# An unused buffer of 1,408 bytes ahead of the streamed buffers of a convolution and two MLPs

## What is computed

```
out  = einsum('hk,bskhg->bshg', softmax(weight), windows(x))   # 7 taps
h    = x @ w_in                                                # MLP 1
g    = where(h >= 1, h, where(h <= -1, 0, (h + 1)**2 / 4))
x    = g @ w_out
h    = x @ moe2_w_in                                           # MLP 2
out  = (h / (1 + exp(-1.702 * h))) @ moe2_w_out
```

## Time and profile before

| What | Value |
|---|---|
| Median of three runs | 1178.54 us |
| The profiled execution, its own time | 1179.53 us |
| Its span (first to last instruction) | 1177.8 us |
| Mean granted clock of TensorE | 0.993 |
| Busy: TensorE, its weight loads | 97%, 87% |
| Busy: VectorE, ScalarE, GpSimd | 70%, 68%, 36% |

### The profile page before, as it was taken

The page is one execution under the profiler, slowest core; times in us unless marked ns, Lnnn a source line. Parts: engine busy times, 40 slices in busy tenths (PEclk is TensorE's granted clock), DMA queues, the critical chain, the costliest instruction groups (busy, mean ns, idle before and its releaser), DMA issues.

```text
span 1177.8 us, 25920 instructions
## 1 busy us (share of the span) xinstructions
PE 1146.4 (97%) x9382; PEld 1021.9 (87%) x9382; DVE 820.4 (70%) x1206; ACT 795.8 (68%) x1510; POOL 429.1 (36%) x425
## 2 busy tenths in 40 slices
PE   7999889999999999999999999999999999999998
PEld 4768679989989999889988999888988988899987
DVE  6877557677676867767677686767767676676633
ACT  4866476776867677686776767677676766765554
POOL 5892909053170714508062260804408062000000
PEclk9999989999999999999999999999999999999999
DMA  6312010001010010100001010010101000000001
GB/s 192 97 40 71 2 35 15 35 3 47 1 48 1 10 40 1 48 1 15 35 5 44 1 48 2 12 37 1 48 1 48 1 7 9 2 15 3 14 1 28
DMA packets 63857, 31.27 MB, mean 27 GB/s; under 512 B 56084, under 2 KB 60562, under 8 KB 63760
## 3 DMA queue, kind: packets, MB, share of 16 engines
q1 hardware_dynamic: 63760, 29.80, 9.5%
HBM read 23.09 MB, written 6.29 MB: 25 GB/s over the span
## 4 chain that ended last, share of the span: by engine, by line
PE 71%; ACT 11%; issue 6%; DVE 6%; POOL 5%; DVEq 0%; ACTq 0%; POOLq 0%
ACT raw L986 3%; ACT clip L936 3%; DVE gate L1103 3%; PE acc_all L748 3%; PE acc_all L762 2%; PE acc_all L754 2%; PE acc_all L757 2%; PE acc_all L759 2%; PE acc_all L765 2%; PE h_all L697 2%; PE h_all L699 2%; PE h_all L701 2%; PE h_all L692 2%; PE h_all L695 2%; PE acc_all L738 2%
## 5 line engine op out<-in xcount | busy, mean ns | idle before, releaser
L1109 DVE TENSOR_TENSOR g_lo<-gate,g_hi 128x512 fp32r<-128x512 f32 x232 | 190.0, 819 | 153.0 <-ACT g_hi L942 153.0
L942 ACT ACTIVATE g_hi<-gate 128x512 fp32r<-128x512 f32 x232 | 146.5, 632 | 201.0 <-DVE gate L1103 199.4
L1115 DVE TENSOR_TENSOR g_lo<-h_all,g_hi 128x512 fp32r<-128x512 f32 x256 | 175.0, 684 | 117.7 <-ACT h_all L953 115.8
L950 ACT ACTIVATE g_hi<-h_all 128x512 fp32r<-128x512 f32 x256 | 152.9, 597 | 87.1 <-PE h_all L703 58.1
L508 POOL TENSOR_TENSOR x_conv<-x_in,tap_w 128x384 f32<-128x384 f32 (+1 forms) x29 | 24.8, 875 | 508.8 <-ACT raw L986 506.5
L936 ACT ACTIVATE clip<-clip,half 128x512 f32<-128x512 f32 x256 | 184.3, 720 | 34.8 <-DVE clip L1094 32.6
L1094 DVE TENSOR_SCALAR clip<-h_all 128x512 f32<-128x512 f32 x256 | 174.8, 683 | 23.5 <-PE h_all L701 19.9
L508 POOL TENSOR_TENSOR prod<-x_in,tap_w 128x384 f32<-128x384 f32 (+1 forms) x174 | 181.2, 1065 | 4.2
L515 POOL TENSOR_TENSOR x_conv<-x_conv,prod 128x384 f32<-128x384 f32 (+1 forms) x174 | 179.8, 1055 | 1.6
L1103 DVE TENSOR_TENSOR gate<-h_all,clip 128x512 f32<-128x512 f32 x232 | 159.3, 687 | 19.5 <-ACT clip L936 8.7
L953 ACT ACTIVATE h_all<-h_all 128x512 f32<-128x512 f32 x256 | 151.6, 592 | 0.1
(11 more groups left out here) (281 smaller groups left out, 4766.0 us busy)
## 6 DMA issues: line engine op xcount, KB each, us to landing
x_in<-in_x SPq DMA_DIRECT2D x14, 960.0 KB, 4.8
out_y<-raw SPq DMA_DIRECT2D x360, 16.0 KB, 1.4
raw<-in_moe_w_out SPq DMA_DIRECT2D x6, 384.0 KB, 4.0
raw<-in_moe_w_in SPq DMA_DIRECT2D x4, 512.0 KB, 3.8
raw<-in_moe_w_in SPq DMA_DIRECT2D x8, 256.0 KB, 4.5
stage<-in_moe_w_out SPq DMA_DIRECT2D x2, 384.0 KB, 7.5
x_in<-in_x SPq DMA_DIRECT2D x1, 768.0 KB, 11.0
x_in<-in_x SPq DMA_DIRECT2D x2, 283.5 KB
```

The lines of the kernel that those rows point to most:

```text
L942: nc.scalar.activation(g1_hi[step.s % G_RING][:, :], gate1_of(step)[:, :], ACT.Copy).then_inc(g1_hi_ready, 1)
L950: nc.scalar.activation(g2_hi[step.s % G_RING][:, :], src, ACT.Gelu_apprx_sigmoid).then_inc(g2_hi_ready, 1)
L1109: nc.vector.tensor_tensor(g1_lo[k][:, :], gate1_of(step)[:, :], g1_hi[k][:, :].bitcast(FP32), ALU.subtract).then_inc(g1_lo_ready, 1)
L1115: nc.vector.tensor_tensor(g2_lo[k][:, :], bank2(step)[:, :], g2_hi[k][:, :].bitcast(FP32), ALU.subtract).then_inc(g2_lo_ready, 1)
```

## The change

A buffer that nothing reads or writes is allocated between x_conv and x_set. Every buffer allocated after it moves up by 352 x 4 = 1,408 bytes; those before it stay. No instruction is added or taken away.

```diff
@@ -80,6 +80,8 @@
         x_blocks = [raw[0][:, 0:TT], raw[0][:, TT:2 * TT]]
         x_turned = [raw[1][:, 0:TT], raw[1][:, TT:2 * TT]]
 
+
+        sb("pad", [P, 352])
         x_set = [[sb(f"x_{k}_{side}", [P, TT], FP32R) for k in ("hi", "lo", "rest")] for side in "ab"]
         y_set = [[sb(f"y_{k}_{side}", [P, TT], FP32R) for k in ("hi", "lo", "rest")] for side in "ab"]
         y_part = sb("y_part", [P, TT])
```

## The result

The changed kernel took 1190.9 us (1190.42 to 1191.46, four runs) against 1178.72 us for the kernel before (1177.29 to 1179.02, four runs). The ratio is 1.0105, 95% interval 1.009 to 1.012: 12.2 us slower, outside the forecast's range and five times what a measurement can tell from nothing. The profiled execution of the changed kernel took 1190.42 us, with a span of 1188.7.

The account below looks back on a forecast made before the run. The prediction took TensorE's matmul rate as the bound. Between a 68 us gain and a 28 us loss it took 0 for the address, and zero for other engines and first loads: 1178.5 us, range 1174.5 to 1181.5 us.

Parts of the forecast that it names:

- What bounds the kernel: Whole kernel: TensorE is busy 97% of the span, so only the rate at which matmuls follow each other matters.
- Where the buffers lie: Streamed x, y and g buffers start 640 above a multiple of 2,048 before and at 0 after; weights stay.
- Rival E: Allocator's origin or order differs from the arithmetic, so the change doesn't do what it says; 1178.5 us, chance inside 0.73.
- the tail's four alignments: Second MLP's last tile: w_down streams at 128, 1,664, 1,152 and 640 above a multiple of 2,048, all 175 ns; taken as 0.
- crossings of 2,048 bytes: Streams read by TensorE: crossing a multiple of 2,048 bytes was taken to cost zero.
- The rule of the skill: Operand starts of 640 and 0 are both multiples of the 16-byte cacheline, so the sum stays at 0.
- rival D: TensorE's matmuls: next weight load runs into this stream, up to 232.5 ns a pair, 28 us slower, 1206 us; chance 0.10.
- Rivals A and B: A: stream's start costs the 13.6 ns, 1111 us, chance 0.06; B: same, but weight loads bind next, 1140 us, chance 0.05.
- the 13.6 ns: Paired matmuls at full clock: time per pair beyond the columns, 226.9 ns against 213.3 ns for 512 columns.
- Rival C: Slots of pairs: only irregular spacings get better, 20 ns x 232 = 5 us faster, 1173.9 us; chance 0.06.
- Other engines: ScalarE and VectorE on the moved buffers: 50 ns a slot at most, inside their free time, so nothing.
- the first loads: Moved stage buffers carrying the first w_out chunks: zero, with 1 us as the bound upwards.

Follow-up runs that it names:

- the maps: Four kernels with the computation left out, only matmuls at one placing of weights and stream after another; 226.7 ns a matmul settled at distance 0.

## Why the prediction was wrong, point by point

- **What bounds the kernel** was right: nothing but the rate of the matmuls moved, and it moved the whole time.
- **Where the buffers lie** was right as far as the runs can tell: the sums of sizes give the distances, and every kernel with another padding came out by them. With the origin of 16,512 that the maps' kernels write down, x_hi of side a lies at 16,512 + 147,968 = 164,480, which is 80 x 2,048 + 640, and the shift makes it 81 x 2,048. No trace shows an address. Rival E is out, since the time moved.
- **The step that failed** is the sentence "Between these ends I take 0, since the tail's four alignments are the nearest rows to the question and differ by nothing". It put the unknown term at nothing, and the runs showed 5.4 ns a pair, 12.2 us, in its place. All four have the weights at the stream's own remainder by 256, distance 0. Rows that vary the alignment by 512, 1,024 and 1,536 are four times the same case, so they spoke on crossings of 2,048 bytes, where they were right (with everything moved the streams cross none, and the time stayed), and on nothing finer. They also stream 384 columns, where the map has a price of 2.7 ns for distance 128 and not 6. The prediction saw that no stream started on a multiple of 512, and still gave the finer rules 0.27 of the chance.
- **The rule of the skill.** The prediction set "SBUF — State Buffer" of the Trainium skill beside its 0: a start's alignment there is a matter of legality, and the cacheline has 16 bytes. The section says that its runs timed nothing, so it never spoke for 0, and the prediction read too much into it. Nor is a line of 16 bytes the unit of the price: in the maps 4 bytes cost 12 ns. The part Who interferes with whom of that page of the Trainium skill was named against rival D. It speaks of ports between engines, and the map agrees that no other engine is needed. It also has stream and weight load on two independent ports; here, all the same, the spacing changed by 6.6 ns with the distance between the two.
- **Rival D** was what happened: it named the place, the distance of 128, the sign, and 0.228 to 0.233 us for a pair, where 0.2314 and 0.2333 were found. Its chance of 0.10 was far too small. The argument against it, that one weight slice in four starts at the streams' 640, failed like the tail's: by 256 all four slices are at distance 0. Its price was over twice the measured one, 28 us against 12.2, because it let all 4,984 matmuls pay and none of the waits shrink. Part pay already: the 232.5 ns after L754 in the earlier trace rows follow no idle time that the trace shows, and in the median the ten acc_all pairs of a slot took 2.299 us before instead of 10 x 226.7 = 2.267. And 10.8 us of weight-load waits were there to be used up; the prediction looked at the matmuls' waits only, the 0.2 us of L740 in the earlier trace rows, where the loads waited 3.6.
- **Rivals A and B** fall: with x, y and g on multiples of 2,048 and the weights moved along, the time is that of before. So the 13.6 ns aren't a head thrown away, and the match of 32 columns with 128 bytes meant nothing.
- **Rival C** came out with the other sign: at the new distance nearly every spacing is longer, the regular ones of h_all too (2.096 us for nine pairs instead of 2.040).
- **Other engines** and **the first loads** at nothing: nothing shows against it. The list of waits of TensorE's matmuls has no new one over 2 us.

## What to carry to other kernels

Where TensorE is the bound and fp32r operands stream in 512 columns, look at the distance between the stationary and the moving operand by 256 bytes before any alignment to a round number: here it costs 1% of the kernel, and a padding that moves one side alone does it by accident. Place both at one remainder (with 320 columns it made no difference, with 448 the other placing was quicker, and other types weren't measured), and after any change to the list of buffers look at the start-to-start distance of the matmuls, since the instruction durations hardly show it (a median of 392 ns against 386). When rows seem to test a rule, write down which variable they really vary: four alignments were one distance.

## What the runs showed that was not expected

At full clock a stream of 512 fp32r columns settles at 226.7 ns at best, 13.3 over the columns, and at 228.9 to 239.0 at nearly all other distances from the weights; at half clock (425 to 427 ns) neither is seen. The Trainium skill ("TensorE: Matmul & The Clock Gate", Wait — 56ns, not 53.3ns?) has about 2.5 ns over the columns for back-to-back matmuls, in a part whose example is bf16; here, in fp32r with a weight load before each, it is 13.3 at 512 columns at best, and for this case the measurement decides. Fewer weight columns make it no better (230.0 ns with 64), and 384 or 320 streamed ones leave the same 13.3. Some distances have more than one settled rhythm: 128 gave 232.6 in one placing and 233.3 in another; -16 bytes gave 226.7 and +240, the same remainder by 256, gave 233.3; -4 gave 228.9 in one run and 231.1 in another on another chip. So the turn of 256 is shown for the multiples of 256 from -256 to 1,792, and open otherwise. What part of the memory or of TensorE makes the turn is open too: the four maps showed the price by address and spoke against the four theories of load and swap (B, F, O, P), and none took their place.
